# A chain of three float32 layers on one core: two weight sums moved on VectorE, GpSimd's first split held back, TensorE's wait moved into the first spatial block

## The reference, cut to what matters

```python
out = einsum('bhsd,bhde->bhse', q, einsum('bhsd,bhse->bhde', k, v))      # attention without softmax, B=8 H=8 S=576 HD=64
x   = out / rms(out) * g_norm                                            # -> (8, 576, 512)
u   = x + (x^T @ U @ V)^T                                                # first mixture: token mixing of rank 32
x2  = u + relu(u @ w_ch1) @ w_ch2                                        # 512 -> 2048 ("up"), 2048 -> 512 ("down")
h   = gelu_tanh(x2 @ w_in)                                               # second mixture: 512 -> 1024
u_, v_ = h[..., :512], h[..., 512:]
v_n = layernorm(v_) * g_ln
v_s = einsum('ts,bsd->btd', w_sg, v_n) + b_sg                            # "spatial" product
y   = x2 + (u_ * v_s) @ w_out
```

## Time and profile before

| | |
|---|---|
| median of 3 runs | 1265.05 us (1261.31 to 1265.84) |
| profiled execution, its own time | 1264.98 us |
| span of its trace | 1263.4 us |
| TensorE busy (matmuls) | 1237.5 us, 98% |
| VectorE, ScalarE, GpSimd busy | 927.5, 575.8, 110.3 us |
| share of TensorE in the chain that ended last | 92% (VectorE 5%) |
| mean granted TensorE clock | 0.997 of full speed |

### The profile page before, as it was taken

How to read it: one execution, slowest core, us unless ns; L and a number is a source line. 1 busy time by engine, 2 the same in 40 slices (tenths; PEclk the granted TensorE clock), 3 DMA queues, 4 the chain that set the end, 5 groups by cost and what they waited for, 6 DMA issues and landing times.

```text
span 1263.4 us, 21859 instructions
## 1 busy us (share of the span) xinstructions
PE 1237.5 (98%) x8129; PEld 1196.5 (95%) x8129; DVE 927.5 (73%) x1380; ACT 575.8 (46%) x942; POOL 110.3 (9%) x123
## 2 busy tenths in 40 slices
PE   7999999999999999999999999999999999999998
PEld 6889999999999999999999999998898998998987
DVE  5987667676757668988888888978765667558564
ACT  4665455554545546554544544544333333343330
POOL 5440000000000000000000000002011211211100
PEclk9999999999999999999999999999999999999999
DMA  9678877888787677473553637371252251350421
GB/s 209 185 201 211 206 200 201 228 207 209 198 216 209 182 240 273 148 261 119 181 174 125 220 112 265 101 211 46 44 107 60 62 125 40 80 117 24 104 59 42
DMA packets 364840, 195.87 MB, mean 155 GB/s; under 512 B 259776, under 2 KB 334800, under 8 KB 364768
## 3 DMA queue, kind: packets, MB, share of 16 engines
q1 hardware_dynamic: 360480, 189.77, 54.1%
q0 software_dynamic: 1728, 4.57, 1.5%
q10 hardware_dynamic: 2560, 0.59, 0.2%
HBM read 118.19 MB, written 74.58 MB: 153 GB/s over the span
## 4 chain that ended last, share of the span: by engine, by line
PE 92%; DVE 5%; issue 1%; DMA 1%; ACT 1%; POOL 1%; ACTq 0%; DVEq 0%
PE ps L1770 28%; PE ps L1772 28%; PE ps L1771 28%; PE ps L1791 2%; PE ps L1802 2%; PE ps L1810 1%; DVE w L1284 1%; PE ps L2085 1%; PE ps L2088 1%; PE ps L1775 1%; PE ps L1828 1%; DMA w_raw<-in_moe_w_ch 1%; PE ps L1804 0%; DVE y L1240 0%; POOL w_raw L797 0%
## 5 line engine op out<-in xcount | busy, mean ns | idle before, releaser
L1770 PE MATMUL ps<-x_hi,w 128*128 128x288 f32 x896 | 268.6, 300 | 3.2 <-DVE h_st L1324 2.1
L1771 PE MATMUL ps<-x_lo,w 128*128 128x288 f32 x896 | 265.0, 296 | 0.0
L1772 PE MATMUL ps<-x_hi,w 128*128 128x288 f32 x896 | 264.8, 296 | 0.0
L1770 PE MATMUL ps<-r_hi,w_hi 128*128 128x384 f32 x672 | 224.6, 334 | 0.3 <-DVE r_lo L1495 0.3
L1772 PE MATMUL ps<-r_hi,w_lo 128*128 128x384 f32 x672 | 224.5, 334 | 0.0
L1771 PE MATMUL ps<-r_lo,w_hi 128*128 128x384 f32 x672 | 224.5, 334 | 0.0
L1089 ACT ACTIVATE r_hi<-hb 128x768 fp32r<-128x768 f32 x168 | 142.3, 848 | 166.4 <-PE ps L1772 161.3
L1770 PEld LDWEIGHTS ps<-x_hi,w 128*128 128x128 f32 x896 | 168.8, 188 | 5.6 <-DVE h_st L1324 2.8
L1772 PEld LDWEIGHTS ps<-x_hi,w 128*128 128x128 f32 x896 | 169.2, 189 | 0.0
L1771 PEld LDWEIGHTS ps<-x_lo,w 128*128 128x128 f32 x896 | 169.1, 189 | 0.0
L1497 DVE TENSOR_TENSOR r_lo<-hb,r_hi 128x768 fp32r<-128x768 f32 x120 | 114.5, 956 | 30.8 <-ACT r_hi L1089 30.8
(11 more groups left out here) (196 smaller groups left out, 2541.6 us busy)
## 6 DMA issues: line engine op xcount, KB each, us to landing
hT_scratch<-h_st SPq DMA_DIRECT2D x64, 576.0 KB, 4.2
hb<-hT_scratch SPq DMA_DIRECT2D x24, 1536.0 KB, 7.2
uT_scratch<-x_raw SPq DMA_DIRECT2D x32, 288.0 KB, 4.7
x_st<-uT_scratch SPq DMA_DIRECT2D x24, 384.0 KB, 3.5
x2T_scratch<-x_st SPq DMA_DIRECT2D x24, 384.0 KB, 5.7
x_raw<-x2T_scratch SPq DMA_DIRECT2D x16, 576.0 KB, 4.0
xt_in<-x2T_scratch SPq DMA_DIRECT2D x144, 64.0 KB, 2.6
y_scratch<-y SPq DMA_DIRECT2D x26, 320.0 KB, 3.1
```

The source lines that it names most:

```text
L1770: mm(dst, ws[0], xs[0], start=first, stop=False, skip_group_check=chained)
L1771: mm(dst, ws[0], xs[1], start=False, stop=False, skip_group_check=chained)
L1772: return mm(dst, ws[1], xs[0], start=False, stop=last, skip_group_check=chained)
```

## The change

Three edits. On VectorE, in the last up tile, `w2_sum(1)` moves from step 19 to step 22, and `w2_sum(3)` from step 36 to step 39. On GpSimd, the first `x2_low` of the second mixture waits also until `s_slo` is 4, that is until VectorE has made the last of `wu_sum_low`. On TensorE, `spatial(0, 0)` starts when four tiles of `ws_lo` are there, and waits for the join of the tails only in front of the first tail matmul.

```diff
-            def x2_low(p, par):
+            def x2_low(p, par, first=False):
                 n = (NJ * P, S)[par]
+                if first:
+                    pool.wait_ge(s_slo, 4)
                 for half in range(2):
...
-            x2_low(0, 1)
+            x2_low(0, 1, first=True)
...
-                    if k in (16, 19, 26, 36):
-                        w2_sum((16, 19, 26, 36).index(k))
+                    if k in (16, 22, 26, 39):
+                        w2_sum((16, 22, 26, 39).index(k))
...
-            def spatial(p, par):
+            def spatial(p, par, first=False):
...
                         for j in range(JM):
                             product(dst, [vn_hi[:, j, cs], vn_lo[:, j, cs]], [ws_hi[:, j, hs], ws_lo[:, j, hs]], j == 0, False)
 
+                        if first and c == 0 and h == 0:
+                            pe.wait_ge(s_wsb, 1)
                         mm(dst, vn_hi[:, JM, cs], ws_lo[:, JM + par, hs], start=False, stop=False)
...
-            pe.wait_ge(s_wsb, 1)
+            pe.wait_ge(s_wslo, JM)
             pe.wait_ge(s_wclo, 3 * DC)
-            spatial(0, 0)
+            spatial(0, 0, first=True)
```

## The result

| | before | changed |
|---|---|---|
| median of 7 runs | 1261.76 us (1260.64 to 1265.84) | 1254.93 us (1254.30 to 1257.36) |
| ratio to before | | 0.9939, 95% interval 0.9926 to 0.9951 |
| profiled execution, own time | 1264.98 us | 1254.60 us |
| span of its trace | 1263.4 us | 1253.0 us |

The change makes the kernel 6.8 us faster by the medians, 0.61% by the ratio (0.49 to 0.74%), which is 7.7 us (6.2 to 9.3). Two of the three runs of before that the prediction had were high: four more bring its median from 1265.05 to 1261.76. The kernel before was run again beside the experiments, in three sets: their medians are 1263.36 (25 runs), 1262.38 (15) and 1263.06 us (11).

What follows compares the result with a forecast made beforehand. TensorE, busy nearly all of the span, was taken as the bound, so only its waits and lower clock could be won. 1.45 + 1.00 + 3.23 + 1.52 = 7.2 us off 1264.98 gave 1257.8 us, range 1254.5 to 1260.8.

Steps and rivals of the forecast that it cites:

- Edit 1, second group: Last up tile, TensorE's wait at step 26: starts near 468.05 instead of 468.72, gain 0.67 us; about 0.9 us stays.
- Edit 1, third group: Last up tile, TensorE's wait at step 40 goes: gain 0.78 us, with about 1.1 us of cover left for the next join.
- The gain lasts: First down tile: the weight quarter's DMA moves along with TensorE, so the up tile's 1.45 us stays whole, bounds 0 and 2.6.
- Case (b): First down tile: the weight quarter does not move, TensorE waits 1.45 us more at 521; gain 5.75, 1259.2 us; chance 0.10.
- case (c): Spatial product: `vs` is late still, TensorE waits about 1 us; 1258.8 to 1260 us; chance 0.10.
- Edit 3: TensorE's wait in front of the first spatial matmul goes: 1.00 us, worth nothing alone because VectorE sets the later wait.
- Edit 2's wait: Spatial product, TensorE's wait for the first `vs` goes once GpSimd's split is held: gain 3.23 us, 0.5 us to spare.
- The clock: Spatial product, two blocks behind the wait for `vs`: without the long wait no fall of the granted clock, gain 1.52 us.
- case (a): Spatial product: the clock's share is not in the difference; gain 5.7, 1259.3 us; chance 0.17.
- What the held split meets: VectorE's gate: two products may be held up to 2 us each; `vs` unaffected, split ends 3.7 us before `v_product`.
- Case (d): Gate: the split is late instead, `v_product` waits 3.8 us, clock falls, VectorE 2.2 us later; 1265.3 us; chance 0.03.
- The chances: Whole kernel: faster by over 0.5% 0.56, within 0.41, slower 0.03.

Runs made afterwards that it cites:

- the run with the other quarter order: Changed kernel with weight sum 1 at step 24, plus another order of the last weight quarters in the first down tile: 1254.41 us, ratio 0.9936.

## Why the prediction was right or wrong

*The difference: right.* Forecast 7.2 us; in the two profiles the change's stretches give 7.1, the medians 6.8, the ratio 7.7 (6.2 to 9.3). The 7.1 hold the clock's 1.5 only because this profile of before had the fall; against the last profile of before, which had none, the same stretches give 5.9. The ratio's interval lies above 5.9, so most of the forecast's 1.5 for the clock, or something else that these profiles do not show, is in the times too.

*The time: 2.9 us too high*, 1257.8 against 1254.93. The step that failed is the base: "The sum is made against the profiled execution", 1264.98 us. I took that it stood at the median of three runs for a sign that it was typical. It was not: before has a median of 1261.76 in the runs beside the change and 1262.38 to 1263.36 in the later sets, so the base was 1.6 to 3.2 us too high. With 1261.76 the same sum gives 1254.6, with the later medians 1255.2 to 1256.2. What the profiled execution had more than others lies in its start. It took 447.2 us up to the last up tile, where eleven of the other thirteen profiles took 443.8 to 444.9. In front of the first matmuls with `y_hl`, at 66 us, it had a distance of 2.78 us, and its granted clock was at the lower level from 67 to 71 us. Eleven profiles, that of the changed kernel among them, have 1.74 to 1.76 us there and no fall, which is 2.6 us less for the wait and the 50 matmuls behind it. The two others that have 2.77 and 2.78 us are the late ones: sum 1 at step 24, without a fall, at 445.96, and the run with the other quarter order, with a fall, at 448.56. What makes that wait longer in some executions stays open.

*Edit 1, second group: right.* 0.67 us forecast, 0.69 measured (1.85 to 1.16), 0.9 us left over. That the rest was due to the weight sum alone was shown by moving it on, to step 24: the rest went.

*Edit 1, third group: right.* Step 40 is on time. The cover in front of the join of step 49 was forecast at 1.1 us and is 1.11.

*The gain lasts: right.* The first down tile's distance is 0.71 us where it was 0.66. The transfers moved with TensorE: ScalarE begins the high half of the late weight quarter at 502.54 us instead of 507.28. Case (b) is out. So is case (c), since `vs` came ahead of need.

*Edit 3: right*, 1.0 us together with edit 2 (0.89 of distance and 0.10 behind it), and nothing alone, as its own run shows.

*Edit 2's wait: right.* 3.23 us forecast. The stretch of blocks 0 and 1 gives 3.24, of which 0.10 belong to edit 3 by the prediction's way of counting, and 0.10 of the forecast lie in the next stretch; `vs` 0.64 us ahead, 0.5 forecast.

*The clock: right in what a fall costs, wrong in counting it whole.* This term of the sum was sized for one execution. 1.52 us is the price of one fall (9.05 or 9.06 against 7.53 in three profiles of before). But the wait of 2.95 us brings it in some executions only, two of four profiles, so on the mean of runs its removal is worth less than 1.52. That was case (a), given 0.17; counted by half, which is an estimate from four profiles, the forecast would have been a gain of 6.4 instead of 7.2. The ratio's interval, 6.2 to 9.3, holds both. How often the clock falls in unprofiled runs was not measured.

*What the held split meets: right in kind.* The gate products took 1.79 and 2.39 us, 1.0 and 1.6 more than the 0.76 of one without a split beside it, under the "up to 2 us" each that was forecast; `vs` was untouched, `v_product` did not wait. Case (d) did not come. Both its parts are real, as the run with the split held longer showed (VectorE's lateness was put at 2.2 us and measured 2.1), but in the changed kernel they stayed out, because the split ended 3.7 us ahead of its user.

*The chances.* Faster by over 0.5% was given 0.56; the ratio is at 0.61%, its interval reaches just across that line.

## What to carry to other kernels

A wait that TensorE has behind VectorE can be GpSimd's doing: look in the timeline for VectorE instructions with two SBUF operands that take several times their usual length (here 2.93 us for 0.38, and 3.12 for 0.69) while GpSimd works, and hold GpSimd's instruction until they are through, but no longer than its own user allows. Move the wait that ends last first; an edit in front of it that does not move its releaser, as edit 3 here, was worth nothing alone. And before a sum is set against one profiled execution, compare the stretches that the change does not touch with other executions, since here the start alone differed by up to 4.8 us from profile to profile (443.8 to 448.6).

## What the runs showed of the hardware that I had not expected

- Behind the same wait of 2.94 to 2.97 us on TensorE the granted clock fell in two profiles and did not in two; the three of the kernel before alone have both kinds. Behind 3.92 us it fell in three of three, once for so long that the two blocks took 9.80 us instead of 7.53. At 66 us, idle times of 2.48 or 2.49 us have both kinds as well: two profiles with a fall behind them, one without.
- Joining two waits of 0.7 and 2.9 us into one of 3.9 us leaves their sum as it was, and with edit 1 in place the kernel was 2.0 us slower by the medians (1262.10 against 1260.09); without edit 1 it was not (1263.17 against 1263.36). The reason is open.
- A difference of 0.43 us in the start of GpSimd's split (873.50 or 873.93 us) decides whether VectorE or the split is held: `wu_lo` took 3.10 or 0.68 us. When the split came 0.16 us behind the start of `wu_lo`, it was the split that waited.
